# Attention, mixture of experts and a last layer on one core: the opening reordered, tile 0's maxima spread from SBUF, the output gates computed tile by tile

## The reference

```python
m_new = np.maximum(f_gate[:, :, t] + m, i_gate[:, :, t])
f_stab = np.exp(f_gate[:, :, t] + m - m_new)
i_stab = np.exp(i_gate[:, :, t] - m_new)
C = f_stab * C + i_stab * np.einsum('bhd,bhe->bhde', vt, kt)
n = f_stab * n + i_stab * kt
h_tilde = np.einsum('bhde,bhe->bhd', C, qt)
denom = np.maximum(np.abs(np.einsum('bhd,bhd->bh', n, qt)), 1.0)
o = 1.0 / (1.0 + np.exp(-o_gate[:, :, t]))
y[:, :, t] = o * h_tilde / denom
```

## Time and profile before

| what | value |
|---|---|
| median of 3 runs | 555.62 us |
| the profiled execution's own time | 555.85 us |
| its span | 554.1 us |
| TensorE busy | 518.5 us (94%) |
| DVE busy | 231.7 us (42%) |
| ACT busy | 133.4 us (24%) |
| GpSimd busy | 103.1 us (19%) |
| chain that ended last | TensorE 89%, DVE 4%, DMA 3%, ACT 2% |
| end of the attention loop's last x_sb | 88.5 us |

### The profile page before, as it was taken

The page is one execution under the profiler, slowest core; times in us unless marked ns, Lnnn a source line. Parts: engine busy times, 40 slices in busy tenths (PEclk is TensorE's granted clock), DMA queues, the critical chain, the costliest instruction groups (busy, mean ns, idle before and its releaser), DMA issues.

```text
span 554.1 us, 8825 instructions
## 1 busy us (share of the span) xinstructions
PE 518.5 (94%) x2735; PEld 352.9 (64%) x2736; DVE 231.7 (42%) x501; ACT 133.4 (24%) x281; POOL 103.1 (19%) x126
## 2 busy tenths in 40 slices
PE   2999994389999999999999999999999999999997
PEld 1889993366666666666566666666666566566664
DVE  6389886741131211212213113121112666666663
ACT  3555543002111111111211211111111223323331
POOL 2535430221011001001004101100004312312100
PEclk9999998599999999999999999999999999999999
DMA  6867844667777674101001001101003111111100
GB/s 206 283 207 239 266 135 153 197 215 237 232 245 204 199 259 149 33 31 52 26 26 52 26 26 52 40 24 40 12 25 95 37 48 47 51 44 47 35 13 36
DMA packets 33220, 60.18 MB, mean 109 GB/s; under 512 B 5600, under 2 KB 22336, under 8 KB 33072
## 3 DMA queue, kind: packets, MB, share of 16 engines
q1 hardware_dynamic: 24768, 42.72, 23.8%
q0 software_dynamic: 3136, 10.03, 6.6%
q10 hardware_dynamic: 5296, 7.17, 3.7%
HBM read 49.96 MB, written 9.95 MB: 108 GB/s over the span
## 4 chain that ended last, share of the span: by engine, by line
PE 89%; DVE 4%; DMA 3%; ACT 2%; issue 1%; POOL 0%; ACTq 0%; DVEq 0%; POOLq 0%
PE ps_y L1208 24%; PE ps_lr L1187 10%; PE ps_y L1267 9%; PE ps_a L1187 9%; PE ps_b L1197 5%; PE ps_y L1126 4%; PE ps_lr L1172 4%; PE ps_a L1253 4%; PE ps_lr L1253 4%; PE ps_a L1172 4%; PE ps_t L1156 3%; PE ps_a L1097 2%; PE ps_b L1276 2%; DMA gate_o<-og 2%; PE ps_lr L1082 2%; PE ps_b L1106 1%
## 5 line engine op out<-in xcount | busy, mean ns | idle before, releaser
L892 DVE COPY hT<-ps_b 128x512 f32<-128x512 f32 x86 | 55.4, 686 | 202.7 <-PE ps_b L1197 182.5
L1208 PE MATMUL ps_y<-w_sb,hT 128*128 x496 | 138.7, 433 | 0.5 <-issue 0.5
L1208 PEld LDWEIGHTS ps_y<-w_sb,hT 128*128 128x128 f32 x496 | 93.1, 190 | 42.8 <-issue 8.4
L504 POOL DMA_INDIRECT xg<-x_dram,token_idx x31 | 29.6, 954 | 238.8 <-PE ps_t L1156 234.7
L1187 PE MATMUL ps_a<-w_sb,xT 128*128 x128 | 57.7, 593 | 0.0
L1187 PE MATMUL ps_lr<-w_sb,xT 128*128 x120 | 55.5, 605 | 0.0
L1267 PE MATMUL ps_y<-wout_sb,hT 128*128 128x320 f32 x192 | 53.8, 433 | 0.9 <-DVE hT L892 0.9
L1267 PEld LDWEIGHTS ps_y<-wout_sb,hT 128*128 128x128 f32 x192 | 35.6, 190 | 15.1 <-issue 1.1
L883 DVE COPY xT<-ps_t 128x384 f32<-128x384 f32 x43 | 23.8, 553 | 48.8 <-PE ps_t L1156 48.8
L619 ACT COPY y_sb<-ps_y 128x320 f32<-128x320 f32 x31 | 13.2, 425 | 122.7 <-PE ps_y L1208 122.7
L1187 PEld LDWEIGHTS ps_lr<-w_sb,xT 128*128 128x128 f32 x120 | 21.6, 189 | 26.5 <-issue 26.5
(11 more groups left out here) (177 smaller groups left out, 567.7 us busy)
## 6 DMA issues: line engine op xcount, KB each, us to landing
w_sb<-w SPq DMA_DIRECT2D x8, 1280.0 KB, 6.3
w_sb<-w SPq DMA_DIRECT2D x16, 512.0 KB, 4.8
mb_sb<-m_dram SPq DMA_DIRECT2D x12, 512.0 KB, 5.4
y_dram<-y_sb ACTq DMA_DIRECT2D x31, 160.0 KB
kvo_sb<-kvo SPq DMA_DIRECT2D x12, 324.0 KB
qk_sb<-qk SPq DMA_DIRECT2D x24, 160.0 KB
w_sb<-w SPq DMA_DIRECT2D x16, 128.0 KB, 5.2
gate_o<-og ACTq DMA_DIRECT2D x1, 1920.0 KB, 8.8
```

What stands on the lines that cost most here:

```text
L504: pool.indirect_dma_start(out=xg[:, b % 2], out_offset=None, in_=x_dram, in_offset=bass.IndirectOffsetOnAxis(ap=token_idx[:, b:b + 1], axis=0)
L892: dve.tensor_copy(hT[:, n * 4:n * 4 + 4], ps_b[:, n].rearrange("p (k s) -> p k s", s=P)).then_inc(ready, 1)
L1208: last = pe.matmul(ps_y[:, 0:DM], hT[:, k], w.rearrange("p o n -> p (o n)"), start=(k == 0), stop=(k == FT - 1))
```

## The change

- SP and ACT issue the loads of the f and i gate rows ahead of their increments. DVE's increments, and the memsets of the PSUM half and of state, go behind the scans and the chunk ends, the memset of nought behind the factor arguments.
- Tile 0's maxima no longer pass through DRAM: eight transfers, four on SP's queue and four on ACT's, spread each head's first 128 maxima from m_row's one partition to the 128 partitions of mb_sb. The stores to m_dram follow on ACT's queue. The load of tile 1's inputs goes ahead of the maxima; GpSimd masks tile 0 before it waits for the factors.
- The sigmoid over all tiles is gone. og comes in three loads, issued by ACT after the factors; ACT takes exp(-o) of one tile after that tile's decays. DVE's finish is tden = (exp(-o) + 1) times the denominator, a reciprocal of tden over 320 columns, and x_sb = yi times tden. The reciprocal over 8 columns at L791 is gone.
- For the first two tiles there is no product with the state (its value is zero), no fading, and copies in place of the two additions; for the last two tiles no keys are scaled, no update is formed and no state is made.

```diff
@@ -318,11 +318,11 @@
 
         @block.sync
         def _(sp):
+            sp.dma_start(f_row[:], gates[0]).then_inc(f_in, 16)
             for s in (*y_out, *s_out):
                 sp.sem_inc(s, 16)
             for s in x_out:
                 sp.sem_inc(s, 32)
-            sp.dma_start(f_row[:], gates[0]).then_inc(f_in, 16)
 
             def load(t, u):
                 for odd in range(2):
@@ -339,16 +339,15 @@
 
             sp.wait_ge(zeroed, 1)
             load(0, 0)
+            load(1, 1)
             sp.wait_ge(gate_rows, 4)
-            for b in range(B):
-                sp.dma_start(m_dram.rearrange("(c b) h s -> b h c s", b=B)[b],
-                             m_row[b * H:(b + 1) * H].rearrange("r (c s) -> r c s", c=NCH)
-                             ).then_inc(m_out, 16)
+            for h in range(0, H, 2):
+                sp.dma_start(mb_sb[:, 0, h], m_row[h:h + 1, 0:P].unsqueeze(1).broadcast_to([1, P, P])).then_inc(mb_in[0], 16)
             sp.wait_ge(m_out, 32)
-            load_mb(0, 0)
             for u in range(1, U):
-                load(u, u)
                 load_mb(u, u)
+                if u + 1 < U:
+                    load(u + 1, u + 1)
...
@@ -380,7 +379,7 @@
             sp.wait_ge(logits_done, done(NT - 1))
 
 
-            sp.wait_ge(rows_set, 1)
+            sp.wait_ge(rows_set, 4)
...
-            pool.sem_inc(state_faded, R)
+            pool.sem_inc(state_faded, R + B)
...
-            pool.wait_ge(turned_copied, 2)
-            pool.wait_ge(factors_ready, 1)
             behind = pool.to_reg(-NEG)
-            for t in range(NT):
-                u = t % U
-                pool.wait_ge(tile_in[u], 48 * (t // U + 1))
-                pool.wait_ge(update_done, done(t - R))
-                pool.tensor_tensor(
-                    kw[:, t % 2], kvo_sb[:, u, H * DV:KVO].rearrange("p (h d) -> p h d", h=H),
-                    factors[:, 0, t].unsqueeze(2).broadcast_to([P, H, D]), ALU.mult).then_inc(kw_ready, 1)
-
-
-                pool.wait_ge(mb_in[u], 16 * (t // U + 1))
+
+            def mask(t, u):
+
+
+                pool.wait_ge(mb_in[u], 16 * (t // U + 1) + (16 * (H - 1) if u == 0 else 0))
                 pool.affine_select(out=mb_sb[:, u], in_=mb_sb[:, u], pattern=[[0, H], [1, P]],
                                    compare_op=ALU.is_ge, fill=behind, base=0, channel_multiplier=-1
                                    ).then_inc(masked, 1)
 
+            mask(0, 0)
+            pool.wait_ge(factors_ready, 1)
+            for t in range(NT):
+                u = t % U
+                if t < NT - B:
+                    pool.wait_ge(tile_in[u], 48 * (t // U + 1))
+                    pool.wait_ge(update_done, done(t - R))
+                    pool.tensor_tensor(
+                        kw[:, t % 2], kvo_sb[:, u, H * DV:KVO].rearrange("p (h d) -> p h d", h=H),
+                        factors[:, 0, t].unsqueeze(2).broadcast_to([P, H, D]), ALU.mult).then_inc(kw_ready, 1)
+
+                if t >= 1:
+                    mask(t, u)
+
+
+                if t < B or t >= NT - B:
+                    continue
...
 
         @block.scalar
         def _(act):
+            act.dma_start(i_row[:], gates[1]).then_inc(i_in, 16)
             for s in (xT_ready, decay_ready, b_ysb, s_exp, s_sq, s_osb):
                 act.sem_inc(s, R)
             act.sem_inc(s_part, R + LEAD)
             act.sem_inc(b_relu, R)
-
-            act.dma_start(i_row[:], gates[1]).then_inc(i_in, 16)
-            act.dma_start(gate_o[:], og).then_inc(og_in, 16)
             act.wait_ge(zeroed, 2)
             for k, (k0, kn) in enumerate(KT):
                 act.dma_start(wgn_sb[0:kn, k, 0:2 * E], wgn[k0:k0 + kn]).then_inc(wgn_in, 16)
             act.dma_start(noise_sb[:], noise).then_inc(small_in, 16)
             act.dma_start(g_sb[:], g_ln).then_inc(small_in, 16)
-            act.wait_ge(og_in, 16)
-            act.activation(gate_o[:], gate_o[:], ACT.Sigmoid).then_inc(sigmoids, 1)
+            act.wait_ge(gate_rows, 4)
+            for h in range(1, H, 2):
+                act.dma_start(mb_sb[:, 0, h], m_row[h:h + 1, 0:P].unsqueeze(1).broadcast_to([1, P, P])).then_inc(mb_in[0], 16)
+            for b in range(B):
+                act.dma_start(m_dram.rearrange("(c b) h s -> b h c s", b=B)[b],
+                              m_row[b * H:(b + 1) * H].rearrange("r (c s) -> r c s", c=NCH)
+                              ).then_inc(m_out, 16)
 
             act.wait_ge(turned_copied, 3)
             act.wait_ge(factor_args, 3)
             act.activation(factors[:], factors[:], ACT.Exp).then_inc(factors_ready, 1)
+            for n in range(3):
+                act.dma_start(gate_o[:, n * U:(n + 1) * U], og[:, n * U:(n + 1) * U]).then_inc(og_in[n], 16)
 
...
+            def gate(t):
+
+                act.wait_ge(og_in[t // U], 16)
+                act.activation(gate_o[:, t], gate_o[:, t], ACT.Exp, scale=-1.0).then_inc(gate_ready, 1)
+
             for t in range(NT):
                 fade(t)
+                gate(t)
...
@@ -690,17 +710,9 @@
                 ins.then_inc(dve_step, 1)
                 dve.wait_ge(dve_step, steps[0])
 
-            for s in (prob_ready, inter_scaled, state_ready, y_ready, x_ready, b_xT, expert_here, b_hT,
-                      s_x2, s_xT, s_max, s_mean, s_centred, s_var, s_vT):
-                dve.sem_inc(s, R)
-
-
             step(dve.memset(keep_row[:], 1.0))
             step(dve.memset(keep_row[:].rearrange("r (c s) -> r c s", c=NCH)[:, :, 0:1], 0.0))
             step(dve.memset(shift_row[:], 0.0))
-            dve.memset(nought[:], 0.0).then_inc(rows_set, 1)
-            dve.memset(state[:], 0.0).then_inc(rows_set, 1)
-            dve.memset(ps_b[:, 1], 0.0).then_inc(rows_set, 1)
             dve.memset(ends_row[:, 0, 0:1], NEG).then_inc(rows_set, 1)
             dve.wait_ge(f_in, 16)
...
-            dve.wait_ge(rows_set, 4)
+            dve.wait_ge(rows_set, 1)
...
                               ).then_inc(gate_rows, 1)
+            dve.memset(ps_b[:, 1], 0.0).then_inc(rows_set, 1)
+            dve.memset(state[:], 0.0).then_inc(rows_set, 1)
+            for s in (prob_ready, y_ready, x_ready, b_xT, expert_here, b_hT, state_ready,
+                      s_x2, s_xT, s_max, s_mean, s_centred, s_var, s_vT):
+                dve.sem_inc(s, R)
+            dve.sem_inc(inter_scaled, R + B)
...
+            dve.memset(nought[:], 0.0).then_inc(rows_set, 1)
             dve.wait_ge(factors_ready, 1)
...
             def finish(t):
 
-                step(dve.tensor_tensor(tden[:], yi[:, t % 2, :, 0:D], den[:].unsqueeze(2).broadcast_to([P, H, D]),
-                                       ALU.mult))
-                dve.wait_ge(sigmoids, 1)
+                dve.wait_ge(gate_ready, t + 1)
+                step(dve.scalar_tensor_tensor(out=tden[:], in0=gate_o[:, t].rearrange("p (h d) -> p h d", h=H),
+                                              scalar=1.0, in1=den[:].unsqueeze(2).broadcast_to([P, H, D]),
+                                              op0=ALU.add, op1=ALU.mult))
+                step(dve.reciprocal(tden[:], tden[:]))
                 dve.wait_ge(x_out[t % U], 32 * (t // U + 1))
                 if t >= U:
                     dve.wait_ge(x_turned, done(t - U))
-                dve.tensor_tensor(x_sb[:, t % U], tden[:].rearrange("p h d -> p (h d)"), gate_o[:, t],
-                                  ALU.mult).then_inc(x_ready, 1)
+                dve.tensor_tensor(x_sb[:, t % U].rearrange("p (h d) -> p h d", h=H), yi[:, t % 2, :, 0:D],
+                                  tden[:], ALU.mult).then_inc(x_ready, 1)
 
             for t in range(NT):
                 weigh(t)
                 if t >= 1:
                     finish(t - 1)
 
-                dve.wait_ge(inter_done, done(t))
-                dve.wait_ge(x_ready, done(t - 2))
-                dve.tensor_tensor(yi[:, t % 2], ps_inter.rearrange("p (h d) -> p h d", h=H),
-                                  factors[:, 1, t].unsqueeze(2).broadcast_to([P, H, DV]), ALU.mult
-                                  ).then_inc(inter_scaled, 1)
-
-                dve.wait_ge(state_faded, done(t))
-                dve.wait_ge(update_done, done(t))
-                dve.tensor_tensor(state[0:KP, t % 2, 0:H], state_f[0:KP, t % 2], update, ALU.add
-                                  ).then_inc(state_ready, 1)
+                if t >= B:
+                    dve.wait_ge(inter_done, done(t))
+                    dve.wait_ge(x_ready, done(t - 2))
+                    dve.tensor_tensor(yi[:, t % 2], ps_inter.rearrange("p (h d) -> p h d", h=H),
+                                      factors[:, 1, t].unsqueeze(2).broadcast_to([P, H, DV]), ALU.mult
+                                      ).then_inc(inter_scaled, 1)
+
+                if t < B:
+                    dve.wait_ge(rows_set, 3)
+                    dve.wait_ge(update_done, done(t))
+                    dve.tensor_copy(state[0:KP, t % 2, 0:H], update).then_inc(state_ready, 1)
```

(36 more changed lines are left out.)

18 lines of the change are left out of this document (2 added, 16 removed).

## The result

The changed kernel takes 582.58 us (median of 4 runs, 580.93 to 584.82) against 555.68 for the kernel before on the same chip (4 runs, 555.32 to 555.8): ratio 1.0482, 95% interval [1.0456, 1.0508], slower by 27 us. The forecast was 577, with a range of 562 to 583. The profiled execution took 582.35 us with a span of 580.3, so it stands for the median. In all that follows a time is the median of all runs of a kernel, and a ratio leaves out runs more than 1.5% over the kernel's fastest: one of x1_dram's four, one of x8_staged's ten, five of x11_warm's twelve.

A forecast was written before the change was run, and what follows sets the result against it. TensorE bound the loop at 5.53 us a tile, DVE hidden at 4.9. Slow maxima (tile 1 at 35.4) and DVE-bound tiles of 6.6 put the loop end 21.1 us later: span 575.2, time 577 us, range 562 to 583.

The forecast's parts named there:

- The scans: Opening on DVE: the scan starts at 3.1 instead of 5.89, a gain of 2.8 us; m_row ready at 7.7.
- the increments (1.15) now stand in front: Opening on DVE: 1.15 us of increments, with two memsets, now precede aT's copy, putting it at 10.6.
- The maxima: Opening: eight 64 KB transfers spreading tile 0's maxima land at 25.3; tile 0's weighting follows at 29.0.
- eight run one after another: Tile 0's maxima: eight transfers taking turns at 2.2 us each, 17.6 us in all, landing at 25.3.
- ACT free at 14.6: Opening on ACT: factors by 12.9 to 13.4, then three og loads issued near 0.4 us each.
- Tile 1 at 35.4: End of the opening: tile 1's weighting at 35.4, after TensorE's late updates, warm-up and value products; before, 27.10.
- rival 1: Opening: fast spread, landing by 12 to 14, tile 1's weighting about 23, 564.5 us; landing at 18, 570. Chance 0.34.
- rival 2: Opening: spread takes 26 us, or og and tiles 2 and 3's loads come late as well; 583 us. Chance 0.06.
- The reciprocal and the loop: Attention loop: reciprocal over 320 elements takes 2.08 us; DVE becomes the bound at 6.6 us a tile, over TensorE's 5.53.
- The end: Loop end: the last x_sb ends at 109.6, 21.1 after 88.54, giving a span of 575.2 us.
- Rival 3: Loop: reciprocal costs 0.5 us, TensorE bounds again; 550.5 with fast spread (chance 0.04), 563 with slow (0.03).
- Rival 4: Loop: removed state products don't take effect; their savings lie under DVE anyway, no change of the sum. No chance given.

The follow-up runs named there:

- x1_dram: Changed kernel with tile 0's maxima taken through DRAM again, nothing else undone: 570.92 us, ratio 1.0224 to the kernel before.
- x8_staged: x6_m0 with og's second and third load issued after the gates of tiles 1 and 3: 557.69 us, ratio 1.002 to the kernel before.
- x11_warm: x6_m0 with tile 0's warm-up products moved ahead of the wait for the weighted keys: 557.43 us, ratio .9975 without its five slowest.
- x4_ports: Changed kernel with heads 0 to 3 on SP's queue and 4 to 7 on ACT's, instead of even and odd: 574.79 us, ratio 1.0357.
- x3_both: Changed kernel with maxima through DRAM and a multiplication by 1 replacing the 320-column reciprocal, which its output lacks: 557.61 us, ratio 1.0033.
- x10_nostate: Kernel before with only the state products dropped where there is no state: 554.27 us, ratio .9991.
- x6_m0: Changed kernel with tile 0's maxima (4 KB) stored to DRAM first and loaded back, gates as tanh, 8-column reciprocal: 556.72 us, ratio 1.0019.
- x7_scans: Kernel before with only the opening's reordering, gate row loads and scans moved to the front: 555.58 us, ratio 1.0004.
- x11_again: x11_warm unchanged, run once more on the same chip as x13_fill: 558.23 us, ratio 1.0036 to the kernel before.
- x12_best: x10_nostate plus x7_scans' scans, x6_m0's small store, early tile 1 inputs and mask, no tile 0 warm-up products: 558.21 us, ratio 1.0068.
- x13_fill: x11_warm with eight more pairs of warm-up products after tile 0's state update: 554.37 us, ratio .9985 to the kernel before.

## Why the prediction was right

**The scans: right.** f_row's issue, 0.7 forecast and 0.80 measured; first memset 1.25 and 1.02; scan 3.1 and 2.89; m_row ready at 7.7 and 7.60. Wrong was what comes next: aT's copy was put at 10.6 and came at 9.56, 0.4 after TensorE had turned a_row and m_row. The term "the increments (1.15) now stand in front" was too dear: behind memsets of 0.48 and 0.67 the fifteen increments cost nothing that can be seen. It was of no weight, since the mask came later.

**The maxima: right in the time, by luck in the row.** Landing at 25.3 was taken between 11.9 and 26; the mask, which waits for it, starts at 26.40, and tile 0's weighting at 30.06 where 29.0 was forecast: 1.1 late. The row chosen for it (48 KB on few partitions, 2.2 us) hit the sum by way of "eight run one after another". Nothing tied that row to this source, and x4_ports shows that the transfers need not take turns: there they move at 57 GB/s. They share a source of 27 GB/s, and the order of the heads kept both queues at one. The estimate of 19 us, drawn in the prediction from the Trainium skill (SBUF — State Buffer, Door 1: The DMA port swizzle) for queues that take turns, is what the run from 7.6 to 26.4 shows.

**ACT free at 14.6: wrong**, the step "factors by 12.9 to 13.4". The issues themselves are held up: four on SP take 9.15 us, four on ACT 7.98, and the two stores behind them 8.33, so ACT gets to its table load at 24.04. It was hidden, with 1.7 us to spare: the mask is ready at 27.5, the factors at 25.8.

**Tile 1 at 35.4: too early by 2.8**, the step "TensorE ... to 32.4, then value products 2.05". TensorE ended its warm-up products at 34.1 and its value products at 35.9, which by the prediction's own steps puts tile 1 at 36.8, 1.4 late. The other 1.4 are a path that the sum did not have: tile 1's maxima are loaded only when m_row's stores have landed, issued 26.71 and masked from 34.57, 7.9 us beside og's 1.9 MB in a stretch with a DMA share of .99. That these maxima set tile 1's weighting stood in rival 1 alone, and late loads behind the spread in rival 2; both belonged into the forecast.

**The reciprocal and the loop: right.** 2.08 forecast, 2.15 measured: from 203 ns at 8 to 2153 at 320 is 6.25 ns an element. DVE is the bound, 6.6 forecast, 6.58 measured, and its stalls, put at 0.5 a tile, are 0.49 by the means of the groups. ACT's exponential takes the 0.45 us said, though not by the reason given: 2.45 us for 1024 would make 0.77 for 320. Tile 1 to tile 2 took 7.3 instead of 6.2, with value products of 2.97 us at a low clock.

**The end: 3.5 us late.** Loop end 109.6 forecast as the end of the last x_sb, 113.1 measured: 2.8 from tile 1, 1.1 from tile 2, 0.4 back in the rest. Left out was the clock behind it: 580.3 - 113.1 is 467.2, before it was 465.6. The 1.6 us lie in the first rows after the loop, which run at .50 and .77 where before's had .59 and .83: the last logits are there 1.0 later after x_sb (six products of 1.59 us in place of 0.91), and the 24 warm-up products take 5.41 us, not 4.80. So 575.2 was forecast for the span and 580.3 came. The 582.58 lie above the forecast's own upper edge of 580. The range of 562 to 583 holds them by 0.4 us, through the part given to rival 2: the main terms were right, the range was met with luck.

**The rivals.** Rival 1 with its landing at 18 was priced at 570; x4_ports, with its mask at 19.35, gave 574.8. Rival 3's combination of a cheap reciprocal and a fast spread was priced at 550.5; x3_both, with its mask at 17.70 and not at 13 to 15, is the nearest case and gave 557.6. Both prices were short by the same things, the loads beside og's and longer warm-up products. (Some of these sums are off by a little: by their own terms 564.5, 570 and 550.5 are 564.3, 569.4 and 550.2.) Rival 4 stood as forecast: in after the dropped products lie under DVE; alone, in x10_nostate, 1.2 us show.

## What to carry to other kernels

Price an elementwise reciprocal by its elements and keep it on the narrow tensor; a gate's own reciprocal over the wide one made a hidden engine the bound. Read one row to all partitions from DRAM, or take the sources from different groups of four partitions in turn, since here one group gave 27 GB/s to two queues and two groups gave 57. And before something is moved to the front of a kernel, look at what its first transfer will then stand behind, and at whether TensorE stays busy in between: here 2.8 us saved on DVE moved the mask by 0.8, since the stores landed behind the same loads as before.

## What was not expected of the hardware

- Issues take long behind a slow source: 2.0 to 4.2 us for each transfer in the mean on SP and ACT, where others take 0.36. The same two stores of m_row take 8.33 us to issue behind the spread and 0.64 in x1_dram. Everything behind them on that engine waits, compute too.
- The low clock makes its own remedy dear. Warm-up products meant to keep the clock up take 4.15 to 5.49 us where they start late, 2.94 before, and then stand in the way of the work (x3_both, x6_m0, x7_scans, x8_staged). A low clock is in the record for x6_m0 and x8_staged (.50); for x3_both and x7_scans the record shows 1.00, so it has gaps or something else slows the products.
- A store of 4 KB takes 3.0 to 3.8 us (x8_staged, x11_again) or 7 (x12_best) until it counts as landed, in step with the end of the traffic issued ahead of it. The slices don't tell whose bytes they are, so that it waits for its turn is inferred, from these runs and the stores of before, x7_scans and x10_nostate.
- Dropping useless products could cost time by the clock alone: x10_nostate's slowest execution has a mean clock of .969, its fastest .981. No run shows that the dropping does it; what x11_again and x13_fill show is that products put into an idle stretch keep the clock.
